# Window attention and two gated MLP stages on one Trainium2 core: the order of the matmuls inside a block product

## The reference, cut to what matters

```python
attn = softmax(mask(q @ k.T / 8)) @ v        # 2 batches, 8 heads, 576 tokens, head 64, window 64
x = attn as [1152, 512]
h = x @ w_in                                  # 512 -> 2048
x = softplus(h) @ w_out                       # 2048 -> 512
p = domain_probs / sum(domain_probs)          # 4 experts
for e in range(4):
    h = maximum(x @ w1[e], 0)                 # 512 -> 1024
    out += p[:, e:e+1] * (h @ w2[e])          # 1024 -> 512
```

## Time and profile before

| | |
|---|---|
| time, median of 3 runs | 633.42 us (632.92 to 633.63) |
| the profiled execution's own time | 633.28 us |
| its span in the profile | 631.5 us |
| PE busy | 621.8 us, 98% of the span, 3880 matmuls |
| PE weight loads busy | 578.4 us, 92%, 3880 loads |
| DVE, ACT, POOL busy | 388.5, 275.9, 86.7 us |
| granted TensorE clock, mean | 0.999 |

### The profile page before, as it was taken

How to read it: one execution, slowest core, us unless ns; L and a number is a source line. 1 busy time by engine, 2 the same in 40 slices (tenths; PEclk the granted TensorE clock), 3 DMA queues, 4 the chain that set the end, 5 groups by cost and what they waited for, 6 DMA issues and landing times.

```text
span 631.5 us, 10128 instructions
## 1 busy us (share of the span) xinstructions
PE 621.8 (98%) x3880; PEld 578.4 (92%) x3880; DVE 388.5 (62%) x867; ACT 275.9 (44%) x634; POOL 86.7 (14%) x84
## 2 busy tenths in 40 slices
PE   7999999999999999999999999999999999999997
PEld 6789999999999999998998998988988988988986
DVE  5987665577645588887267277276276376376342
ACT  5887755556544465552342342332332432432410
POOL 1453333323332332000000000000000000000000
PEclk9999999999999999999999999999999999999999
DMA  8915130023200010023102103003003003000012
GB/s 329 366 42 199 70 134 1 28 106 134 67 2 0 2 34 31 3 67 101 35 0 101 34 1 102 33 1 109 26 1 120 15 1 131 4 0 1 2 51 100
DMA packets 11584, 40.78 MB, mean 65 GB/s; under 512 B 2320, under 2 KB 2320, under 8 KB 10256
## 3 DMA queue, kind: packets, MB, share of 16 engines
q1 hardware_dynamic: 11536, 40.13, 18.1%
HBM read 37.77 MB, written 2.36 MB: 64 GB/s over the span
## 4 chain that ended last, share of the span: by engine, by line
PE 95%; DMA 1%; DVE 1%; ACT 1%; POOL 1%; issue 0%; SPq 0%; DVEq 0%
PE banks L1062 31%; PE banks L1049 28%; PE banks L1018 16%; PE banks L998 16%; PE banks L959 2%; DMA raw_b<-in_w_out 1%; PE banks L985 1%; PE banks L972 1%; PE banks L1068 1%; ACT prob L462 1%; DVE prob L660 0%; POOL wa_lo L427 0%; DVE prob L646 0%; DVE wb_lo L634 0%; POOL sp_c L423 0%
## 5 line engine op out<-in xcount | busy, mean ns | idle before, releaser
L1062 PE MATMUL banks<-wb_hi,ehid_hi 128*128 128x512 f32 x288 | 112.1, 389 | 0.0
L1062 PE MATMUL banks<-wb_lo,ehid_hi 128*128 128x512 f32 x288 | 112.1, 389 | 0.0
L1062 PE MATMUL banks<-wb_hi,ehid_lo 128*128 128x512 f32 x288 | 112.0, 389 | 0.0
L423 POOL TENSOR_TENSOR sp_c<-sp_e,sp_c 128x384 f32<-128x384 f32 x48 | 64.2, 1338 | 134.9 <-DVE sp_c L676 134.9
L810 DVE SCALAR_TENSOR_TENSOR part<-banks,gate,part 128x512 f32<-128x512 f32 x63 | 47.3, 751 | 55.9 <-PE banks L1062 55.9
L1049 PE MATMUL banks<-T_lo,aop_hi 128*128 128x288 f32 x256 | 75.6, 295 | 0.0
L1049 PE MATMUL banks<-T_hi,aop_lo 128*128 128x288 f32 x256 | 75.6, 295 | 0.0
L1049 PE MATMUL banks<-T_hi,aop_hi 128*128 128x288 f32 x256 | 75.3, 294 | 0.0
L998 PE MATMUL banks<-xy_hi,wa_hi 128*128 128x384 f32 x192 | 66.3, 345 | 0.0
L1018 PE MATMUL banks<-hid_hi,wb_hi 128*128 128x384 f32 x192 | 65.8, 343 | 0.1
L1062 PEld LDWEIGHTS banks<-wb_hi,ehid_lo 128*128 128x128 f32 x288 | 54.1, 188 | 11.2
(11 more groups left out here) (98 smaller groups left out, 1233.6 us busy)
## 6 DMA issues: line engine op xcount, KB each, us to landing
unit_in<-in_units SPq DMA_DIRECT2D x8, 1024.0 KB, 7.7
raw_a<-in_w SPq DMA_DIRECT2D x16, 512.0 KB, 3.3
raw_b<-in_w SPq DMA_DIRECT2D x16, 512.0 KB, 3.3
raw_a<-in_w_in SPq DMA_DIRECT2D x8, 512.0 KB, 5.2
raw_b<-in_w_out SPq DMA_DIRECT2D x8, 512.0 KB, 4.2
out_dram<-part SPq DMA_DIRECT2D x9, 256.0 KB, 2.0
part<-in_units SPq DMA_DIRECT2D x2, 1024.0 KB, 12.4
unit_in<-in_units SPq DMA_DIRECT2D x2, 384.0 KB, 6.5
```

What stands on the lines that cost most here:

```text
L423: pool.tensor_tensor(sp_c[:, s, :], sp_e[:, s, :], sp_c[:, s, :], ALU.subtract).then_inc(lost_done, 1)
L1062: m = pe.matmul(TOKEN_BANKS[T], ehid[x][:, i, P * T:P * T + P], wb[a][:, f, :], start=(i == 0 and j == 0), stop=(i == 3 and j == 2))
```

## The change

The three loops around the matmul of `product` are put in another order. Before, the part `s` (the bank) is the outer loop: six matmuls go to the first bank of the pair and then six to the second. After, `s` is the inner loop: the two matmuls with the same stationary half and k-tile follow each other, one to each bank. The same 12 matmuls are issued, with the same operands, the same flags and the same order of additions inside each bank. The stationary operand, in order, is before hi, hi, lo of k=0, hi, hi, lo of k=1, and all of that again; after it is four times hi, twice lo of k=0, then four times hi, twice lo of k=1. Waits and the semaphore at the end stay as they are.

```diff
-                for s in range(2):
-                    for k in range(2):
-                        for j, (a, b) in enumerate(TERMS):
+                for k in range(2):
+                    for j, (a, b) in enumerate(TERMS):
+                        for s in range(2):
                             m = pe.matmul(into[:, s, :], aop[a][:, i, row, k, :], bop[name][b][:, k, HC * s:HC * s + HC],
                                           start=(fresh and k == 0 and j == 0), stop=(k == 1 and j == 2),
                                           skip_group_check=not fresh)
```

## The result

The changed kernel takes 634.44 us (median of 20 runs, 633.85 to 634.90), the kernel before, in the same comparison, 633.59 us (20 runs, 632.92 to 634.16): 0.85 us more, ratio 1.0013 with a 95% interval of 1.0007 to 1.0019. The forecast was no change, 633.4 us. It is a small, real loss, and the forecast of no change did not see it.

A forecast was written before the change was run, and what follows sets the result against it. PE was taken as the bound; repeats and bank changes were priced at zero, so 633.28 + 0 = 633.3, forecast 633.4 us as no change. Range 632.0 to 635.3 us.

The forecast's parts named there:

- PE is the bound, and a nanosecond per matmul goes straight to the end: Third stage: PE is busy for 98% of the span and waits for nobody; products take 178.4 us for 1344 matmuls.
- A repeated stationary tile costs and saves nothing: Block products: four more repeats per call priced at nothing; bounds 5.7 us less or 0.8 us loss.
- The rival of cheaper repeats: Block products: repeated tile spares part of the 13 ns gap; 5.7 us less, 627.7 us; chance 0.12, whole or in part.
- its form with both conditions at once: Saving needs repeated tile and other bank together; all 8 repeats count, 11.4 us, so 622.0; within the shared chance 0.12.
- A bank change costs nothing: Block products: 1120 more bank changes priced at 0, bounds 3.4 us either way.
- The slower rival, dearer bank changes: Block products: each added bank change costs 1.7 ns, 1.9 us in all, so 635.3 us; chance 0.15.
- the bound of 3 ns: Limit per bank change, from two MLP lines with four changes against one, both 2.08 us for 12 matmuls.
- Where the operands lie: Block products: moving address jumps 288 columns each matmul, not each six; -1.4 or +0.8 us, kept as width only.
- the halves at 0.79 and 0.80 us: One product call before the change: six matmuls to the first bank took 0.79 us, six to the second 0.80.
- the width of the forecast: Uncertainty around no change, -1.4 to +0.8 us, if all products cost 131.7 or 133.3 ns.
- A nearly constant 13 ns per matmul: PE, all lines: time beyond the columns at 2.4 GHz, 12.7 ns for products, 13.3 and 13.4 for other lines.
- The clock: PE's clock might fall through gaps from going round banks; 658 or 830 us; chance 0.01.

The follow-up runs named there:

- e3: Kernel before with only the stationary tiles in the order of after, moving operands and banks as before; product stretch of 168 matmuls 22.30 us, as before.
- e1: Kernel before with only the banks alternating as after, stationary and moving operands as before; product stretch of 168 matmuls 22.30 us, as before.
- e2: Kernel before with only the moving operands in the order of after, stationary tiles and banks as before; product stretch 22.38 us against 22.30.
- f2: Kernel before with moving operands read from column 0, widths 256 to 320 by half-expert; time per matmul beyond its columns 10.0 to 13.3 ns.
- The sweep: Kernel before with one start column per half-expert for all moving operands; columns 0, 16, 24 cheap, 8, 28, 32, 40, 48, 56 dear; column 0 took 22.118 us.

## Why the prediction was wrong

- *PE is the bound, and a nanosecond per matmul goes straight to the end.* Right: 0.5 ns on each of 1344 matmuls, with the token stretches behind them, is 0.82 us from the first product to the last token matmul, and the medians moved by 0.85 us.
- *A repeated stationary tile costs and saves nothing.* Right, shown by e3: 22.30 us with eight repeats per call. Loads and matmuls stay 3880 each. The rival of cheaper repeats is dead, also in its form with both conditions at once: e1 has repeats that go to another bank and takes 22.30 us, and the changed kernel has eight per call and is no faster than e2, which has none of that kind.
- *A bank change costs nothing.* Right, shown by e1. The slower rival, dearer bank changes at 635.3, had the sign of the result but the wrong mechanism. The hint that I gave for it, a single step of 0.14 us at a bank change, was mostly rounding: averaged over the 98 calls, that step is 134.8 ns, but the dearest of the 12, 138.1 ns, lies inside a bank, and in e1, with a bank change at every step, the same two are 133.7 and 137.9. The price had a slip as well: half of the bound of 3 ns is 1.5 ns and not 1.7, so 1.7 us and 635.1.
- *Where the operands lie* is the step that failed. I had seen the halves at 0.79 and 0.80 us, had named the address of the moving operand as what might lie behind it, and had worked out what it would be if all matmuls took the dearer value, +0.8 us. Then I used this as the width of the forecast around zero and not as an effect with a sign. The result is that term, near its dear end: all 12 matmuls of a call cost nearly what those of the second half did, 133.2 against 133.3 ns, and the products took 0.66 us more where the term had +0.8. This width reached only to 634.2 us; that 634.44 still lies in my range is owed to its upper end, 635.3, which came from the price of bank changes and so from something that costs nothing. That part is luck. What the runs put in its place: the cost of a matmul depends on where its moving operand and its neighbours' start within 256 bytes, and an alternation of an unlike pair of places is not the mean of the two (22.26 would be the mean; alternating gives 22.38, six by six 22.30).
- *A nearly constant 13 ns per matmul.* The averages of the earlier trace rows did say 12.7 for the products and 13.3 and 13.4 for the other lines. I had the 0.6 ns between them as a bound and priced it at nothing; over 1344 matmuls it is 0.8 us, and the change lost 0.5 ns of it. f2 shows that this part is 10.0 to 13.3 ns by width.
- *The clock.* Right: its level did not change in any slice.

What stays open is why a start place is cheap or dear. The sweep shows which ones are, but no rule, and how neighbours act on each other has none either. I have not shown whether the read of the operand, its hand-over to the array or something else holds the step back.

## What to carry to other kernels

Where PE is dense from end to end, read its step from the length of whole stretches, and treat a difference of half a nanosecond between lines as a fact to be explained: times a thousand matmuls it is the result. Reordering matmuls reorders their reads; where the moving slices start at unlike places within 256 bytes (here slices of 288 columns), try the order together with the place, since the same edit lost 0.85 us at one and gained 2.04 us at another. A profile with another rule in each repetition of a stage settles seven such questions in one run.

## What the runs showed of the hardware

- In a dense stretch a matmul of 288 columns took from 131.3 ns (22.05 / 168) to 133.3 ns (22.40 / 168), by the start places of the moving operands and their order. At the places of the kernel before, the order of the banks and of the stationary tiles had no effect (22.30 us each).
- From one start, 264 columns took 20.16 us for 168 where 256 took 20.15: eight columns for nothing; 272 took 21.05.
- A place's effect carries over into the next stretch: the 108 token matmuls behind the products took 24.49 us behind the order of before, 24.50 behind that of after, and 24.53 behind the reads from column 0, with no instruction of theirs changed.
